# Attention and feed-forward on one core: the start of the kernel rearranged over four engines

## The reference

```python
def rotate(x):
    x1, x2 = (x[..., :half], x[..., half:])
    return np.concatenate([x1 * cos - x2 * sin, x1 * sin + x2 * cos], axis=-1)
q_rot, k_rot = (rotate(q), rotate(k))
scores = scale * np.matmul(q_rot, k_rot.transpose(0, 1, 3, 2))
scores = scores - np.max(scores, axis=-1, keepdims=True)
attn = np.exp(scores)
attn = attn / (np.sum(attn, axis=-1, keepdims=True) + 1e-09)
out = np.matmul(attn, v)
...
h = x @ w_in          # x: 2304 tokens by 512, w_in 512 by 2048
g = np.maximum(h, 0.0) + alpha * np.minimum(h, 0.0)
return g @ w_out      # 2048 by 512
```

## Time and profile before

| | |
|---|---|
| median of 3 runs | 700.78 us (700.7 to 700.98) |
| profiled execution | 700.88 us |
| its span | 699.1 us |
| TensorE busy | 676.6 us, 97% of the span |
| VectorE busy | 372.4 us, 53% |
| ScalarE busy | 314.2 us, 45% |
| GpSimd busy | 282.1 us, 40% |
| DMA | 51.30 MB, SyncE's queue only |

### The profile page before, as it was taken

The page is one execution under the profiler, slowest core; times in us unless marked ns, Lnnn a source line. Parts: engine busy times, 40 slices in busy tenths (PEclk is TensorE's granted clock), DMA queues, the critical chain, the costliest instruction groups (busy, mean ns, idle before and its releaser), DMA issues.

```text
span 699.1 us, 12111 instructions
## 1 busy us (share of the span) xinstructions
PE 676.6 (97%) x4100; PEld 588.0 (84%) x4100; DVE 372.4 (53%) x681; ACT 314.2 (45%) x740; POOL 282.1 (40%) x258
## 2 busy tenths in 40 slices
PE   3899999999999999899999999999999999999996
PEld 3788888888888887698889999999999999999995
DVE  4688888888888878445642333233233323432231
ACT  2777777777777776333332222322322232223222
POOL 6655777777776504122222222222222222222221
PEclk9999999999999999999999999999999999999999
DMA  6897656666666642600001000000000010001001
GB/s 154 220 225 195 147 135 140 142 146 143 143 143 145 148 106 79 239 1 0 1 1 46 0 1 16 31 0 1 30 15 0 0 43 2 0 0 46 2 0 46
DMA packets 76619, 51.30 MB, mean 73 GB/s; under 512 B 61088, under 2 KB 61472, under 8 KB 76064
## 3 DMA queue, kind: packets, MB, share of 16 engines
q1 hardware_dynamic: 76576, 50.76, 28.9%
HBM read 22.95 MB, written 4.72 MB: 40 GB/s over the span
## 4 chain that ended last, share of the span: by engine, by line
PE 76%; issue 16%; POOL 2%; DVE 2%; DMA 1%; ACT 1%; SPq 1%; POOLq 0%; DVEq 0%; ACTq 0%
PE banks L620 19%; PE banks L647 19%; PE banks L547 14%; PE banks L505 12%; PE banks L566 10%; POOL g_lo L449 2%; PE banks L562 2%; DVE nmax L846 1%; DMA k_two<-k_hi 0%; DMA cos_sb<-in_cos 0%; DMA out<-stage 0%; DVE pt L895 0%; DVE k_lo L871 0%; ACT stage L807 0%; SPq L294 0%
## 5 line engine op out<-in xcount | busy, mean ns | idle before, releaser
L449 POOL TENSOR_TENSOR g_lo<-g,g_hi 128x384 fp32r<-128x384 f32 x96 | 99.3, 1035 | 312.2 <-ACT g_hi L795 306.1
L960 DVE TENSOR_SCALAR g<-banks,alpha_sb 128x384 f32<-128x384 f32 x96 | 59.3, 618 | 249.1 <-ACT pos L787 249.1
L620 PE MATMUL banks<-x_hi,w_in_lo 128*128 128x384 f32 x384 | 129.3, 337 | 0.0
L620 PE MATMUL banks<-x_hi,w_in_hi 128*128 128x384 f32 x384 | 129.2, 336 | 0.0
L620 PE MATMUL banks<-x_lo,w_in_hi 128*128 128x384 f32 x384 | 129.0, 336 | 0.0
L787 ACT ACTIVATE pos<-banks 128x384 f32<-128x384 f32 x96 | 47.1, 491 | 169.1 <-PE banks L620 169.1
L846 DVE TENSOR_REDUCE nmax<-banks 128x1 f32<-128x576 f32 x144 | 108.6, 755 | 22.8 <-PE banks L505 17.6
L647 PE MATMUL banks<-w_out_hi,g_hi 128*128 128x512 f32 x288 | 114.9, 399 | 1.6 <-POOL g_lo L449 1.4
L647 PE MATMUL banks<-w_out_hi,g_lo 128*128 128x512 f32 x288 | 112.9, 392 | 0.0
L647 PE MATMUL banks<-w_out_lo,g_hi 128*128 128x512 f32 x288 | 111.9, 389 | 0.0
L795 ACT ACTIVATE g_hi<-g 128x384 fp32r<-128x384 f32 x96 | 50.5, 526 | 119.7 <-DVE g L963 119.7
(11 more groups left out here) (83 smaller groups left out, 909.8 us busy)
## 6 DMA issues: line engine op xcount, KB each, us to landing
k_two<-k_hi SPq DMA_DIRECT2D x64, 160.0 KB, 2.9
out<-stage SPq DMA_DIRECT2D x18, 256.0 KB, 2.0
raw_q<-in_q SPq DMA_DIRECT2D x32, 128.0 KB, 2.8
raw_k<-in_k SPq DMA_DIRECT2D x32, 128.0 KB, 2.4
q_two<-q_hi SPq DMA_DIRECT2D x32, 128.0 KB, 2.3
q_two<-q_lo SPq DMA_DIRECT2D x32, 128.0 KB, 2.3
q_own<-q_hi SPq DMA_DIRECT2D x32, 128.0 KB, 2.4
raw_v<-in_v SPq DMA_DIRECT2D x32, 128.0 KB, 2.3
```

Of the source, the lines that this page charges most:

```text
L449: nc.gpsimd.tensor_tensor(g_lo[f % 2][:, :], g[f % 2][:, :], g_hi[f % 2][:, :].bitcast(F32), ALU.subtract).then_inc(g_lo_done, 1)
L620: mm = nc.tensor.matmul(h_ps[f % 2], w[:, j, cols], xx[:, j, :], start=(step == 0), stop=(step == 3 * CT - 1))
L960: nc.vector.tensor_scalar(g[f % 2][:, :], h_ps[f % 2], 0.0, alpha_sb[:, f:f + 1], ALU.min, ALU.mult).then_inc(neg_done, 1)
```

## The change

- SyncE no longer issues sin, cos and the identity; ScalarE does, before everything else it does. ScalarE also issues two of the four copies into `k_two[0]`, behind the high parts.
- VectorE first clears a 128x128 corner of `prob`, and TensorE multiplies it with itself into PSUM bank 7, which nothing else uses so early: 16 times before it waits for the identity, three times between the turn of the queries and that of the keys, six times behind the last turn.
- The keys' two sine products of the first pair run on GpSimd, counted by a new semaphore `first_swap`. VectorE's order becomes: sine products of the queries, cosine product and sum of the queries, cosine product and sum of the keys. `first_step` has six counts instead of eight.
- Of GpSimd's 14 memsets, four (those of `raw_v[1]` and `q_own[1]`) move behind the sine products. VectorE and ScalarE wait for the first few memsets only.
- `FIRST_TILES` takes in tile 3, and ScalarE waits for that tile before it overwrites `q_hi`.

```diff
--- before.py
+++ after.py
@@ -15,7 +15,7 @@
 REM_TILE, A_TILES, B_TILES = 0, (1, 2, 3, 4), (5, 6, 7, 8)
 TILES = 9
-FIRST_TILES = (1, 2)
+FIRST_TILES = (1, 2, 3)
 U_KQREM, U_QREM = 0, 1
 U_KREM = 2
@@ -48,7 +48,7 @@
     assert 2 * D == P and 2 * REM == P and CT == PAIRS and NCHUNK * CHUNK == TOK and NCHUNK % 2 == 0
     PERIODS = NB * PAIRS
-    PADDED = 15
+    PADDED = 14
     W_COLS = F // (2 * PAIRS)
     W_LAST = F // 4
     Q_STACKED, K_STACKED = 6 * 16, 4 * 16
@@ -213,6 +213,8 @@
         padded = sem("padded")
         rope_step = sem("rope_step")
         first_step = sem("first_step")
+        first_swap = sem("first_swap")
+        blank_done = sem("blank_done")
         q_two_in, k_two_in = sem("q_two_in"), sem("k_two_in")
         scored = sem("scored")
         max_done = sem("max_done")
@@ -266,13 +268,24 @@
             return isinstance(i, int) and i * 2 + c == NCHUNK - 1
+        def first_halves(eng, unit, side, step):
+
+            raw4 = (raw_q, raw_k)[side][:, :, :].rearrange("p t (h d) -> p t h d", h=2)
+            halves = prob[:, side, 0:ST * P].rearrange("p (t h d) -> p t h d", t=ST, h=2)
+            for a, z in ((0, D // 2), (D // 2, 0)):
+                unit.tensor_tensor(halves[:, :, :, a:a + D // 2], raw4[:, :, :, z:z + D // 2],
+                                   sin_sb[:, :, a:a + D // 2].unsqueeze(2).to_broadcast([P, ST, 2, D // 2]),
+                                   ALU.mult).then_inc(step, 1)
+
         @block.sync
         def _(sp):
             def load(p, side):
                 src, raw, landed = ((q_h, raw_q, q_in), (k_h, raw_k, k_in))[side]
                 if isinstance(p, int) and p == 1:
-                    sp.wait_ge(first_step, side * 4 + 3)
+                    sp.wait_ge(first_step, 3 if side == 0 else 5)
+                    if side == 1:
+                        sp.wait_ge(first_swap, 2)
                 elif has_prev(p):
                     sp.wait_ge(rope_step, (p - 1) * 8 + side * 4 + 3)
                 for h in range(2):
@@ -310,17 +323,16 @@
                     sp.dma_start(raw[h * REM:(h + 1) * REM, QT, h * D:(h + 1) * D],
                                  v_h[head + h, QT * P:S, :]).then_inc(v_in, 16)
-            sp.dma_start(sin_sb[:, :, :], sin).then_inc(sin_in, 16)
             load(0, 0)
-            sp.dma_start(cos_sb[:, :, :], cos).then_inc(cos_in, 16)
             load(0, 1)
-            sp.dma_start(ident[:, :], eye).then_inc(ident_in, 16)
             sp.dma_start(alpha_sb[:, :], alpha).then_inc(alpha_in, 16)
-
             load(1, 0)
             load(1, 1)
             stack(0, 0, 0)
-            stack(0, 0, 1)
+            sp.wait_ge(evac[U_K % T_BANKS], evac_count(-1, U_K))
+            sp.wait_ge(evac[U_MIXED % T_BANKS], evac_count(-1, U_MIXED))
+            for head, own, other in ((0, slice(0, D), slice(D, P)), (1, slice(D, P), slice(0, D))):
+                sp.dma_start(k_two[0][own, head, :].bitcast(F32), k_hi[0][own, :].bitcast(F32)).then_inc(k_two_in, 16)
             def batch(b):
                 for t in range(PAIRS):
@@ -403,17 +415,28 @@
             for raw in (raw_q, raw_k):
                 nc.gpsimd.memset(raw[REM:P, QT, :], 0.0).then_inc(padded, 1)
-            for raw in raw_v:
+            for raw in raw_v[0:1]:
                 nc.gpsimd.memset(raw[REM:P, QT, 0:D], 0.0).then_inc(padded, 1)
                 nc.gpsimd.memset(raw[0:REM, QT, D:P], 0.0).then_inc(padded, 1)
             for qrem in (qrem_hi, qrem_lo):
                 nc.gpsimd.memset(qrem[0:REM, REM:P].bitcast(F32), 0.0).then_inc(padded, 1)
                 nc.gpsimd.memset(qrem[REM:P, 0:REM].bitcast(F32), 0.0).then_inc(padded, 1)
-            for own in q_own:
+            for own in q_own[0:1]:
+                nc.gpsimd.memset(own[D:P, 0, :].bitcast(F32), 0.0).then_inc(padded, 1)
+                nc.gpsimd.memset(own[0:D, 1, :].bitcast(F32), 0.0).then_inc(padded, 1)
+            pool.wait_ge(padded, 10)
+            pool.wait_ge(sin_in, 16)
+            pool.wait_ge(k_in, 48)
+            first_halves(pool, nc.gpsimd, 1, first_swap)
+            pool.wait_ge(first_swap, 2)
+            for raw in raw_v[1:2]:
+                nc.gpsimd.memset(raw[REM:P, QT, 0:D], 0.0).then_inc(padded, 1)
+                nc.gpsimd.memset(raw[0:REM, QT, D:P], 0.0).then_inc(padded, 1)
+            for own in q_own[1:2]:
                 nc.gpsimd.memset(own[D:P, 0, :].bitcast(F32), 0.0).then_inc(padded, 1)
                 nc.gpsimd.memset(own[0:D, 1, :].bitcast(F32), 0.0).then_inc(padded, 1)
             pool.wait_ge(padded, PADDED)
-            pool.wait_ge(sin_in, 16)
+            pool.wait_ge(blank_done, 2)
             pool.wait_ge(cos_in, 16)
             rope(1, 0)
@@ -470,7 +493,7 @@
             def turned_in(p, side):
                 if isinstance(p, int) and p == -1:
-                    pe.wait_ge(first_step, side * 4 + 4)
+                    pe.wait_ge(first_step, (4, 6)[side])
                 else:
                     pe.wait_ge(rope_step, (p + 1) * 8 + side * 4 + 4)
@@ -660,9 +683,19 @@
                 if is_final(i, c):
                     output(i, c, FT - 1)
+            def run_in(count):
+
+                for _ in range(count):
+                    nc.tensor.matmul(banks[:, 7, 0:P], prob[:, QT - 1, 0:P], prob[:, QT - 1, 0:P], start=True, stop=True)
+
+            pe.wait_ge(blank_done, 1)
+            run_in(16)
             pe.wait_ge(ident_in, 16)
-            for u in (*OF_NEXT, U_MIXED):
-                turn(-1, -1, u)
+            turn(-1, -1, U_Q)
+            run_in(3)
+            turn(-1, -1, U_K)
+            turn(-1, -1, U_MIXED)
+            run_in(6)
             pe.wait_ge(padded, PADDED)
             def batch(b):
@@ -706,6 +739,8 @@
                 if u == U_Q:
                     if not (isinstance(p, int) and p < 0):
                         act.wait_ge(q_two_in, (p + 1) * Q_STACKED)
+                    if isinstance(p, int) and p == 0:
+                        act.wait_ge(scored, FIRST_TILES[-1] + 1)
                     jobs = [(q_hi[:, :], bank, SCALE)]
                 elif u == U_K:
                     jobs = [(k_hi[(t + 1) % 2][:, REM:S], bank, 1.0)]
@@ -807,11 +842,18 @@
                 nc.scalar.activation(stage[(c * MT + m) % 2][:, :], y_ps[c % 2][m], ACT.Copy).then_inc(staged, 1)
             HEADS = (slice(0, D), slice(D, P))
-            act.wait_ge(padded, PADDED)
+            act.dma_start(sin_sb[:, :, :], sin).then_inc(sin_in, 16)
+            act.dma_start(cos_sb[:, :, :], cos).then_inc(cos_in, 16)
+            act.dma_start(ident[:, :], eye).then_inc(ident_in, 16)
+            act.wait_ge(padded, 4)
             nc.scalar.activation(prob_rem[REM:P, 0:1], raw_v[0][REM:P, QT, 0:1], ACT.Exp)
             for u in (*OF_NEXT, U_MIXED):
                 hi(-1, u, -1)
+            act.wait_ge(evac[U_K % T_BANKS], evac_count(-1, U_K))
+            act.wait_ge(evac[U_MIXED % T_BANKS], evac_count(-1, U_MIXED))
+            for head, own, other in ((0, slice(0, D), slice(D, P)), (1, slice(D, P), slice(0, D))):
+                act.dma_start(k_two[0][other, head, :].bitcast(F32), k_hi[0][own, :].bitcast(F32)).then_inc(k_two_in, 16)
             def batch(b):
                 for t in range(PAIRS):
@@ -1004,24 +1046,24 @@
                 maxima(p, t, B_TILES[3])
                 normalise(p, *before, 1)
-            nc.vector.memset(zero[:, :], 0.0).then_inc(padded, 1)
-            dve.wait_ge(padded, PADDED)
+            nc.vector.memset(prob[:, QT - 1, 0:P], 0.0).then_inc(blank_done, 1)
+            nc.vector.memset(zero[:, :], 0.0).then_inc(blank_done, 1)
+            dve.wait_ge(padded, 2)
             dve.wait_ge(sin_in, 16)
-            for side, (raw, rot, landed) in enumerate(((raw_q, rot_q, q_in), (raw_k, rot_k, k_in))):
-                halves = prob[:, side, 0:ST * P].rearrange("p (t h d) -> p t h d", t=ST, h=2)
+            dve.wait_ge(q_in, 48)
+            first_halves(dve, nc.vector, 0, first_step)
+            dve.wait_ge(cos_in, 16)
+            for side, (raw, rot) in enumerate(((raw_q, rot_q), (raw_k, rot_k))):
                 raw4 = raw[:, :, :].rearrange("p t (h d) -> p t h d", h=2)
                 rot4 = rot[:, :, :].rearrange("p t (h d) -> p t h d", h=2)
-                dve.wait_ge(landed, 48)
-                for a, z in ((0, D // 2), (D // 2, 0)):
-                    nc.vector.tensor_tensor(
-                        halves[:, :, :, a:a + D // 2], raw4[:, :, :, z:z + D // 2],
-                        sin_sb[:, :, a:a + D // 2].unsqueeze(2).to_broadcast([P, ST, 2, D // 2]),
-                        ALU.mult).then_inc(first_step, 1)
-                if side == 0:
-                    dve.wait_ge(cos_in, 16)
+                halves = prob[:, side, 0:ST * P].rearrange("p (t h d) -> p t h d", t=ST, h=2)
+                if side == 1:
+                    dve.wait_ge(k_in, 48)
                 nc.vector.tensor_tensor(rot4, raw4, cos_sb[:, :, :].unsqueeze(2).to_broadcast([P, ST, 2, D]),
```

(4 more changed lines are left out.)

## The result

| | before | changed |
|---|---|---|
| median | 700.79 us (6 runs) | 703.01 us (702.75 to 704.45, 6 runs) |
| ratio | | 1.0032, 95% interval 1.0022 to 1.0042 |
| profiled execution, span | 700.88, 699.1 us | 703.11, 701.3 us |

What follows compares the result with a forecast made beforehand. SyncE's DMA queue was taken to bound the start, setting 32.26. Two issues fewer (-1.25) and the start of `load(1, 1)` (+0.01) gave -1.24 from 700.88: 699.65, forecast 699.6 us, range 698.4 to 701.5.

Steps and rivals of the forecast that it cites:

- pair score: Start of the second pair's first stacked score on TensorE, 32.26 in the old kernel; forecast at 31.0.
- Bound of the old kernel: The number of DMAs on SyncE's queue, 33 issues at 0.625 us each, sets the score at 32.26.
- Start of `load(1, 1)`: SyncE's queue, after the keys' cosine product: `load(1, 1)` starts at 9.17 against 9.16, +0.01 us.
- loads from two queues: sin, cos and identity leave SyncE for ScalarE: VectorE begins at 4.6 instead of 4.78, bounds 4.3 and 5.4.
- Two issues fewer: Two `k_two` copies of the first pair move from SyncE to ScalarE: -1.25 us, bounds 1.25 and 0.
- Landing of the last copy: Last `k_two` copy before the score at 32.26 took 2.96 us to land in the old kernel.
- Sine products on GpSimd: VectorE and GpSimd take turns on two-input SBUF operations, so handing over the keys' sine products brings nearly nothing.
- The clock: Blanks raise TensorE's clock, first score near 12.7; a fall before 19.8 costs about 1 us, with 1.3 to spare.
- a gain that is gone by 32.26 is gone for good: From 32.26 up to 60 us the chain is TensorE back to back; moving 32.26 moves the end one for one.
- Rival C: Blanks on TensorE do not raise the clock and stand in the way: priced at 702.5 us, chance 0.12.
- Third first tile: Six matmuls for four on TensorE cost 0.25 us inside idle time before the score at 32.26: nothing.

Runs made afterwards that it cites:

- h: Old kernel with two of the first pair's four `k_two` copies issued by ScalarE; 700.00 us, ratio 0.9982.
- j: Old kernel with sin, cos and the identity issued by ScalarE instead of SyncE; 702.00 us, ratio 1.0018.
- e3: Changed kernel without its 25 blank products; 702.02 us, ratio 1.0012.
- e4: Changed kernel, whole, with extra blank products in the first period as well; 703.65 us, ratio 1.0034.
- e1: Changed kernel with sin, cos and the identity issued by SyncE again, in the old order; 702.32 us, ratio 1.0016.
- i: Changed kernel with sin, cos and identity loads on SyncE and the keys' sine products on VectorE again; 701.79 us, ratio 1.0013.
- e2: Changed kernel with the first pair's key sine products on VectorE again; 702.05 us, ratio 1.0012.
- k: Changed kernel with loads on SyncE and key sine products on VectorE again, plus blanks in the first period; 702.07 us, ratio 1.0003.

## Why the prediction was wrong

The sum had one path, SyncE's queue, and that path still released the pair score. What failed are its terms. It let the last `k_two` copy issue at 27.92 (29.16 + 0.01 - 1.25) and land 2.96 us later; it issued at 29.73 and landed after 4.00. Of the 2.85 us between 31.0 and 33.86, 1.27 lie in the start of `load(1, 1)`, 0.54 in the two issues fewer, and 1.04 in the landing.

- *Bound of the old kernel:* right. h moved the pair score by 0.56 us and the time by 0.18%.
- *Start of `load(1, 1)`, put at +0.01:* this step failed, and it is the largest. It rests on *loads from two queues*, put at 4.60 with bounds of 4.3 and 5.4, measured 5.96, and 5.86 in j. I had let 224 KB at most go ahead of the queries; in fact each of the transfers in flight took 3.0 to 4.0 us to land instead of 2.2 to 2.9. The Trainium skill, "DMA: Bandwidth & Descriptors", "Issuing engines are not separate DMA queues", says that DMAs of different issuing engines share the 16 DMA engines and interleave, and j agrees. It says too that a second issuing engine saves only the time of issuing; measured, the part is a loss (+1.1 us at VectorE's start).
- *Two issues fewer, put at -1.25:* mis-sized. They saved 0.69 us in h and 0.71 in the changed kernel, since SyncE's issues beside ScalarE's took longer.
- *Landing of the last copy, left at 2.96:* 4.00 us. Nothing in the prediction speaks of it; an `instruction` packet moved beside it, and the cause is open. In e3, with the same issue time and no such packet, it is 3.12.
- *Sine products on GpSimd:* the turns were right, both in kind and in size (1.37 and 1.49 us measured, 1.4 worked out). What followed from them was not followed to the end: with late keys and four memsets behind the products the rope began at 11.40, not 10.05, and GpSimd is the chain from 6.97 to 21.15.
- *The clock:* that a fall costs about 1 us on a path with spare time, and so nothing, failed as a mechanism. The first score started at 14.70, not 12.7. The fall came at 19.6, before TensorE's wait for `rot_k` had begun, lasted 10.2 us, and with a GpSimd chain 1.35 us late it brought TensorE to the pair score at 33.73 instead of 29.7. But it did not set that score alone: `k_two` came 0.13 us behind. e4, where the clock held and TensorE waited 2.5 us, has the same score (its last copy issued 1.0 us later and landed 1.0 us faster).
- *"a gain that is gone by 32.26 is gone for good", and one for one:* nearly. 1.6 of the 2.2 us lie ahead of 33.86. 0.6 us arise in the third period, from the same exclusion of VectorE and GpSimd that rows 10 show, at a copy that the change doesn't touch. I had used the rule for the new code alone.
- *Rival C* was on the right side for a wrong reason. The blanks did raise the clock (32 passes in 6.16 us, where 7.4 would be the slow pace); it fell again.
- *Third first tile:* its two matmuls more lay at 19 to 20.3, partly slow, in front of TensorE's wait of 0.9 us for `rot_k`: free, as said.

How the 2.2 us divide over the parts is not settled: undoing the loads, the sine products or the blanks gives back 0.16, 0.20 and 0.20% of the 0.32%, more in sum than there is, since they share one chain and two paths end together; their intervals overlap.

## What to carry to other kernels

Find the path that sets the end of the start-up phase and count what is queued on it; here two copies taken off SyncE's queue brought 0.2%, while undoing the blanks for TensorE's clock, or the arithmetic handed to GpSimd, won time. When a new chain reaches the point that a queue used to set, look whether the queue is late too: here both ended within 0.13 us, and taking away the delay of one alone showed little (33.70 in e1, 33.89 in e4). A load that is first wanted should be alone on the DMA engines: earlier issue of others is not free. And when an engine is made faster ahead of a wait that stays, look at what its longer idle time triggers.

## What the runs showed of the hardware

- The granted clock in a page stands at full from 0 to the first fall. In the old kernel and in h and j it reads 1.00 throughout the first 60 us, though rows up to some 23 us had half the pace. Only falls after a rise show, as 0.50 in the changed kernel. The pace of the rows is the safer view at the start of a kernel.
- After a fall, half speed lasted 10.2 us (changed kernel, 19.6 to 29.85) and 13.7 us (i, 15.2 to 28.9), with TensorE at work for most of it, but only 3.4 us in e2 and e4 behind the pair score. The same list of instructions up to period 0 gave a fall at 15.2 in i and none in k, which differs ahead of it only by three blanks; whether that varies from run to run of one kernel, as the two groups of k's times suggest, was not seen in a profile.
- A VectorE copy with one SBUF input (`inv_sb`) was held up by GpSimd as well: 0.42 us alone, 1.77 at worst, and it ended 0.28 to 0.29 us behind GpSimd's product in three periods. The Trainium skill, "SBUF — State Buffer", "Who interferes with whom", says that a copy can contend with GpSimd when its operands allow the mode with two ports; the trace agrees that this one does.
- Of SyncE's `k_two` copies of the first pair, the one that took longest to issue took 0.79 to 0.95 us in the twelve kernels where ScalarE issued two others just before, 0.60 in the old kernel and in j.
